# Attention products of a three-stage kernel: from high/low f32r pairs to plain f32 matmuls on 64-row and 64/32-column tiles of the array

## What is computed

```python
def phi(x):                                     # q and k, per head
    proj = x @ w_phi                            # 64 -> 128 features
    proj = proj - max(abs(proj), axis=-1)
    return concatenate([exp(proj), exp(-proj)])
kv, z = phi(k).T @ v, sum(phi(k), over tokens)
x = (phi(q) @ kv) / (phi(q) @ z + 1e-6)         # attention, no softmax matrix

xk, xr = mu_k*x + (1-mu_k)*x_prev, mu_r*x + (1-mu_r)*x_prev
y = sigmoid(xr @ w_r) * (relu(xk @ w_k)**2 @ w_v)          # "moe"

h = relu(y @ w_in)
out = (h * sigmoid(conv3(h))) @ w_out                      # "moe2"
```

## Time and profile before

| | us |
|---|---|
| median of 3 runs | 1486.46 (1486.41 to 1493.02) |
| profiled execution, first to last instruction (its span) | 1483.8 |
| TensorE matmuls busy | 1416.3 (95%) |
| VectorE busy / ScalarE busy | 818.5 / 797.9 (55% / 54%) |
| attention of the first batch, alone | 0 to 118 |
| seven iterations, attention with second stage | 118 to 997 |
| last second stage | 997 to 1057 |
| phase 2 | 1057 to 1484 |

### The profile page before, as it was taken

How to read it: one execution, slowest core, us unless ns; L and a number is a source line. 1 busy time by engine, 2 the same in 40 slices (tenths; PEclk the granted TensorE clock), 3 DMA queues, 4 the chain that set the end, 5 groups by cost and what they waited for, 6 DMA issues and landing times. The chain is left out here.

```text
span 1483.8 us, 26980 instructions
## 1 busy us (share of the span) xinstructions
PE 1416.3 (95%) x10240; PEld 1362.4 (92%) x10240; DVE 818.5 (55%) x1141; ACT 797.9 (54%) x1400; POOL 14.4 (1%) x20
## 2 busy tenths in 40 slices
PE   5778999999999999999999999999889999999998
PEld 5778999999999999999999999999879889988997
DVE  4565555554645564465555555554386468456653
ACT  4656674674666557466565746755244344344442
POOL 0000000000000000000000000000110000000000
PEclk9999999999999999999999999999999999999999
DMA  4412202211120221212122022121201110110101
GB/s 125 126 31 57 58 17 65 69 30 50 45 61 26 57 61 30 66 41 49 38 61 58 17 66 66 27 91 46 72 34 61 68 40 22 67 60 16 51 28 36
DMA packets 153461, 77.42 MB, mean 52 GB/s; under 512 B 131728, under 2 KB 140048, under 8 KB 152336
## 3 DMA queue, kind: packets, MB, share of 16 engines
q1 hardware_dynamic: 153360, 75.91, 18.5%
HBM read 56.71 MB, written 19.02 MB: 51 GB/s over the span
## 5 line engine op out<-in xcount | busy, mean ns | idle before, releaser
L512 PE MATMUL psm<-xk_hi,wk_hi 128*128 128x288 f32 x512 | 153.4, 300 | 16.5 <-DVE xk_lo L885 12.0
L1047 PE MATMUL psh<-y_hi,win_hi 128*128 128x288 f32 x512 | 154.0, 301 | 13.5 <-ACT h L1132 9.1
L1048 PE MATMUL psh<-y_lo,win_hi 128*128 128x288 f32 x512 | 152.5, 298 | 0.0
L512 PE MATMUL psm<-k_hi,wv_hi 128*128 128x288 f32 x512 | 152.1, 297 | 0.0
L1049 PE MATMUL psh<-y_hi,win_lo 128*128 128x288 f32 x512 | 151.9, 297 | 0.0
L512 PE MATMUL psm<-xk_lo,wk_hi 128*128 128x288 f32 x512 | 151.7, 296 | 0.0
L512 PE MATMUL psm<-xk_hi,wk_lo 128*128 128x288 f32 x512 | 151.2, 295 | 0.0
L512 PE MATMUL psm<-k_lo,wv_hi 128*128 128x288 f32 x512 | 151.1, 295 | 0.0
L512 PE MATMUL psm<-k_hi,wv_lo 128*128 128x288 f32 x512 | 150.8, 295 | 0.0
L890 DVE TENSOR_TENSOR k_lo<-square,k_hi 128x288 fp32r<-128x288 f32 x128 | 58.6, 458 | 156.1 <-ACT square L740 155.6
L1190 DVE SCALAR_TENSOR_TENSOR conv<-h,taps,conv 128x576 f32<-128x576 f32 x64 | 55.2, 863 | 141.7 <-ACT conv L1134 141.7
(11 more groups left out here) (157 smaller groups left out, 3832.2 us busy)
## 6 DMA issues: line engine op xcount, KB each, us to landing
den<-den_scr SPq DMA_DIRECT2D x64, 144.0 KB, 3.0
y_scr<-y SPq DMA_DIRECT2D x64, 144.0 KB, 2.6
y<-y_scr SPq DMA_DIRECT2D x8, 1152.0 KB, 5.7
qk_nat<-in_q SPq DMA_DIRECT2D x64, 128.0 KB, 2.5
qk_nat<-in_k SPq DMA_DIRECT2D x64, 128.0 KB, 2.5
v_nat<-in_v SPq DMA_DIRECT2D x64, 128.0 KB, 2.5
out<-rows SPq DMA_DIRECT2D x32, 256.0 KB, 2.0
stage<-in_moe_w_in SPq DMA_DIRECT2D x4, 512.0 KB, 3.2
```

What stands on the lines that cost most here:

```text
L512: return nc.tensor.matmul(o, lhsT, rhs, start=first, stop=last)
L1047: nc.tensor.matmul(o, wh, xh, start=first, stop=False, skip_group_check=True)
L1048: nc.tensor.matmul(o, wh, xl, start=False, stop=False, skip_group_check=True)
```

## The change

The host now lays out q and k transposed (128 rows of two heads, 576 tokens) and v by token block. The step `T`, all splits of attention operands and the diagonal weight block are gone. The products of the attention take plain `F32` operands that cover a part of the array:

- `QP`, `KP`: 64 rows, one head each: 10 matmuls, 128 feature columns. The heads alternate, heads 0 and 1 on rows 0 to 63 and 64 to 127.
- `P0`, `P1` replace `PA`, `PB`: one half of the tokens for both heads: 2 plain matmuls of 64 rows over 288 columns, then 2 f32r matmuls of 64 rows for the maxima.
- `KV`: the same 20 matmuls, 65 columns. One copy out instead of four.
- `DEN` (new): the denominators apart, 8 matmuls with a single stationary column, on PSUM rows 0, 32, 64 and 96.
- `NUM` replaces `NA`, `NB`: 8 matmuls with 64 stationary columns, head 0 on PSUM rows 0 to 63, head 1 on 64 to 127.
- The denominators go out by four DMAs instead of one, and VectorE adds their two parts before it inverts them.

```diff
-PE_NS = {"T": 1100, "QP": 1600, "KP": 1600, "M": 500, "PA": 1000, "PB": 1000, "KV": 2200, "NA": 1500,
-         "NB": 1500, "K": 1480, "K-": 1110, "K+": 370, "R": 1480, "V-": 1480, "V": 1480}
+PE_NS = {"QP": 1100, "KP": 1100, "M": 550, "P0": 800, "P1": 800, "KV": 2240, "DEN": 1000, "NUM": 1950,
+         "K": 1590, "K-": 1190, "K+": 400, "R": 1590, "V-": 1590, "V": 1590}
-FILL_NS = {"QP": 1500, "M": 1500, "PA": 3000, "T": 2200}
+FILL_NS = {"QP": 2200, "M": 1600, "P0": 3500, "P1": 2600}
...
+        steps += [(s, p) for s in ("KP", "M", "EK", "P0", "KV", "P1", "DEN", "NUM")]
+        steps += [("QP", p + 1)] if p + 1 < PAIRS else []
...
         def project(i, p, a):
...
+            for n in range(TT):
+                for h, t in ((0, (n - 1) % TT), (1, (n + 1) % TT)):
+                    own, b = slice(D * h, D * h + D), place(h, t)
...
+                    last = mm(ps[:, F * b:F * b + F], qk[own, p % 2, i, P * t:P * t + P], phi[own, :], True, True)
...
+        def feature_rows(n, p, a):
...
+            for h in range(2):
+                own = slice(D * h, D * h + D)
+                mm(ps1[:, BANK * h:BANK * h + HALF], phi[own, :], qk[own, p % 2, 0, cols], True, False)
+            for h in range(2):
+                own = slice(D * h, D * h + D)
+                last = mm(ps1[:, BANK * h:BANK * h + HALF], pick[own, :], max_rows[own, cols], False, True)
...
+        def sum_den(p, a):
...
+            for n in range(2):
+                cols = slice(HALF * n, HALF * n + HALF)
+                for h in range(2):
+                    for e in range(2):
+                        row = 32 * (2 * h + e)
+                        last = mm(ps[row:row + 1, BANK * (1 + n):BANK * (1 + n) + HALF], kvz[:, h, e, D:D + 1], q_exp[:, e, h, cols],
+                                  True, True)
...
+        def attend(p, a):
...
+            for n in range(2):
+                cols = slice(HALF * n, HALF * n + HALF)
                 for e in range(2):
+                    for h in range(2):
+                        last = mm(ps1[D * h:D * h + D, BANK * n:BANK * n + HALF], kvz[:, h, e, 0:D], q_exp[:, e, h, cols],
+                                  e == 0, e == 1)
```

More of the change, by code:

```diff
@@ L80, in before @@
             return [(s, p - 1)] if p else []
[L82 to L88, removed]
+        steps += [("M", p)] + before("RC") + [("P0", p), ("EK", p)] + ahead("QP")
+        steps += [("KV", p), ("P1", p)] + before("DV") + ahead("KP") + [("DEN", p), ("NUM", p)]
+        if last:
+            steps += [("XK", 2, 0), ("HK", 2, 0), ("LK", 2, 0), ("RC", p)]
+            steps += [("XR", 2, 0), ("HR", 2, 0), ("LR", 2, 0), ("DV", p)]
     return steps + [(s + w, 2, 1) for w in "KR" for s in "XHL"]
@@ L138, in iteration @@
             s, p = step[:2]
-            if not (ran_ahead and step in (("T", 0), ("QP", 0), ("KP", 0))):
+            if not (ran_ahead and step in (("QP", 0), ("KP", 0))):
                 emit(step)
@@ L356, in await_bank @@
         if before < 0 and first_of(batch):
[L357 removed]
+            eng.wait_ge(den_copied, PAIRS)
             return
@@ L386, in load_qk @@
         def load_qk(p, a):
-            await_(sp, turned, PAIRS, a, p)
             reg, off = a
-            for i, (src, loaded) in enumerate(((q, q_loaded), (k, k_loaded))):
-                b = src[off] if reg is None else src[reg + off]
-                for h in range(2):
-                    sp.dma_start(qk_nat[:, i, 0:4, D * h:D * h + D],
-                                 b[2 * p + h, 0:4 * P, :].rearrange("(t s) d -> s t d", s=P)).then_inc(loaded, 16)
-                sp.dma_start(qk_nat[0:TAIL, i, 4, :].rearrange("s (h d) -> s h d", h=2),
-                             b[2 * p:2 * p + 2, 4 * P:S, :].rearrange("h s d -> s h d")).then_inc(loaded, 16)
+            await_(sp, features, H, a, 2 * (p - 1))
+            sp.dma_start(qk[:, p % 2, 0, 0:S], q[off, p] if reg is None else q[reg + off, p]).then_inc(q_loaded[p % 2], 16)
+            await_(sp, k_projected, PAIRS, a, p - 1)
+            sp.dma_start(qk[:, p % 2, 1, 0:S], k[off, p] if reg is None else k[reg + off, p]).then_inc(k_loaded[p % 2], 16)
         def load_v(p, a):
@@ L498, in _ @@
                                 pattern=[[-1, P]], channel_multiplier=1).then_inc(ident_ready, 1)
-        for n, (part, h) in enumerate([(0, 0), (0, 1), (1, 0), (1, 1)]):
+        for n, row in enumerate((0, 1, D, D + 1)):
             pool.wait_ge(pick_made, 1 + n)
-            nc.gpsimd.affine_select(out=pick_f[:, h, :], in_=pick_f[:, h, :], compare_op=ALU.not_equal, fill=-1.0,
-                                    base=-(2 * part + h), pattern=[[0, F]], channel_multiplier=1).then_inc(pick_made, 1)
+            nc.gpsimd.affine_select(out=pick_f, in_=pick_f, compare_op=ALU.not_equal, fill=-1.0,
+                                    base=-row, pattern=[[0, F]], channel_multiplier=1).then_inc(pick_made, 1)
         pool.wait_ge(zeroed, 1)
@@ L592, in attend @@
                 for e in range(2):
-                    last = three(ps1[:, BANK * n:BANK * n + HALF], (kvz_hi[:, h, e, :], kvz_lo[:, h, e, :]),
-                                 (hi[:, e, cols], lo[:, e, cols]), e == 0, e == 1)
+                    for h in range(2):
+                        last = mm(ps1[D * h:D * h + D, BANK * n:BANK * n + HALF], kvz[:, h, e, 0:D], q_exp[:, e, h, cols],
+                                  e == 0, e == 1)
             last.then_inc(attended, 1)
@@ L723, in copy_num @@
[L723 to L730 removed]
+            await_(act, attended, PAIRS, a, p)
@@ L749, in split_mix @@
                 await_(act, r_done, 2 * XT, m, XT * n)
-            if which and n == 2 and m[0] is None and m[1] == -1:
-                act.wait_ge(attended, H)
             await_(act, mixed, 2 * XT, m, XT * n + fs.stop)
```

325 lines of the change are left out of this document (126 added, 199 removed).

## The result

| | before | after |
|---|---|---|
| median of the runs, us | 1486.62 (1486.41 to 1493.02, 4 runs) | 1419.55 (1415.0 to 1425.01, 4 runs) |
| span of the profiled execution, us | 1483.8 | 1415.8 |
| first batch alone, until the second stage's long stretch | 118.3 | 102.9 |
| one iteration, mean of seven | 125.6 | 118.2 |
| last second stage and phase 2 | 486.3 | 485.8 |

A forecast was written before the change was run, and what follows sets the result against it. Seven iterations were taken as bound by TensorE's matmul stream, the first batch by a chain of hand-overs. Sum: 1486.5 - 39 + 18 - 13 + 5 = 1457.5, stated as 1457 us; range 1388 to 1522, the forecast's own 1445 to 1472.

The forecast's parts named there:

- parts replaced, 28 pairs, if tiles cost what their records need: Attention steps on TensorE in the iterations: 8.6 us a pair against 10.0, 39 us less over 28 pairs.
- changes of form in the iterations: TensorE switching between whole-array and partial-tile matmuls: 294 times at 0.06 us, 18 us more.
- new waits in the iterations: `KP` waiting for maxima, `DEN` for exponentials: 0.25 us at three places in each iteration, 5 us more.
- first batch: Attention running alone at the start: earlier start and shorter hand-over chain, less its changes of form, 13 us less.
- Pairs of neighbours overlap, never more, whatever the number of tiles: Tiled attention steps on TensorE: overlap only in pairs, so `DEN` and `NUM` 2.2 us each, 8.6 us a pair.
- first rival: Tiled steps: records queued for one tile don't hold up another; 6.4 us a pair instead of 8.6, 1392 us; chance 0.22.
- The estimate of 1.3 us for `DEN` by that page: `DEN`: its 3.9 us of records divided by the skill's four-row-tile factor 3.07, giving 1.3 us.
- second rival: All 336 changes of form empty the array: 0.23 us each instead of 0.06, 57 us more, 1514 us; chance 0.25.
- The nearest row taken for the price: Trace's plain-to-f32r change after `KV`, 0.06 us more than the pace, taken as the price of a change of form.
- The price of a plain record: Plain f32 matmul records on TensorE: 0.245 us for 288 columns, 0.11 us for 128.
- `KV` paced by its loads: `KV`: weight loads of 128 columns, two for each product, set its pace; one column less changes nothing.
- Work taken off ScalarE and VectorE buys nothing: Seven iterations: the matmul stream is the bound, so removing six large splits a pair gains nothing there.

The follow-up runs named there:

- experiment 1: Changed kernel with `QP`, `KP`, `DEN` and `NUM` issuing all products of one tile, then all of the next, instead of alternating: 1510.0 us, ratio 1.0154.
- experiment 2: Changed kernel with one of twelve f32r matmuls in each of the 64 second-stage tiles `R` covering only 64 rows: 1442.05 us, ratio 0.9697.
- experiment 6: Changed kernel with `KV`'s 128 stationary columns in two pieces of 64, each on its own column tile: 1367.82 us, ratio 0.9197.
- experiment 4: Changed kernel with three useless splits a pair added back, ScalarE copy and VectorE difference waiting for each other: 1468.53 us, ratio 0.9883.
- experiment 5: Same useless operations as experiment 4 on the changed kernel, but ScalarE and VectorE not waiting for each other: 1443.08 us, ratio 0.9705.
- experiment 7: Changed kernel with `KV`'s 128 stationary columns in four pieces of 32, each on its own column tile: 1384.94 us, ratio 0.9321.
- experiment 8: Changed kernel with the first batch's weight-piece loads issued ahead of the loads of q and k: 1424.66 us, ratio 0.9580.
- experiment 10: Changed kernel with `KV` in pieces of 64, weight pieces loaded ahead of q and k and hung on `QP`, `P1`, `NUM`: 1362.21 us, ratio 0.9161.

## Why the prediction came out less than half as large

The direction held and the time lies in the range, but the forecast's own range, 1445 to 1472, missed it. Term by term, in us; measured values are sums over the starts of the two traces (the long stretch holds the projections and transposes of 27 pairs and the other steps of 28; 9.86, 7.35 and 6.30 are its sums shared out over 28):

| term | forecast | measured |
|---|---|---|
| parts replaced, 28 pairs, if tiles cost what their records need | -39 | 28 x (9.86 - 6.30) = -100 |
| changes of form in the iterations | +18 | +50 |
| new waits in the iterations | +5 | -2 |
| first batch | -13 | -15.5 |
| the rest | 0 | -0.5 |

- **The step that failed is the overlap.** "Pairs of neighbours overlap, never more, whatever the number of tiles" was derived from the order of the records. `DEN` alone refutes it: 1.08 us, not 2.2, which is 31 us over 28 pairs. The two-tile steps do not pay a start slot either: `NUM` is 2.09 us for eight slots of 0.242, which is 1.94, and a change. That their whole times, changes included, still came out near the forecast's (`NUM` 2.09 for 2.2, a projection 1.31 for 1.21, `P0` 0.82 for 0.87) is luck: the slot stood in for a change of form that was priced too low. The first rival, "each tile keeps its own order", had 6.4 us a pair for this, and `DEN` at 1.0. Experiment 1 shows how far it goes, to about four records of a tile.
- **The Trainium skill** (TensorE: Matmul & The Clock Gate, Part 3) has matmuls start and end in program order. The trace disagrees for the starts of different tiles: in experiment 1 a later record of one tile starts before earlier queued ones of the other. The estimate of 1.3 us for `DEN` by that page was nearer than the forecast, and still above the 1.08; its factor of 3.07 is one for four row tiles, and `DEN` runs on four column tiles.
- **Changes of form were under-priced as well**, with the opposite sign. The 50 us are 29 inside the tiled steps (28 x (7.35 - 6.30)), 4 in `KV` and the maxima and 16 in the second stage: 0.17 us for each of 294, where 0.06 was taken. Experiment 2 gives 0.20 for 64-row tiles. This is the second rival's mechanism near its upper price. It stayed on the fast side since the first rival came true too: 1392 + 336 x 0.11 is 1429, and 1422 without the 7 us of waits that did not come, near the 1419.6 measured. The nearest row taken for the price, from plain to f32r, was no change of form at all; in the other direction such a change of type costs nothing (302.38 to 302.51). The Trainium skill (TensorEngine Tiling, Key Properties) says that a change of the tiling mode drains the engine. The trace agrees that a change has a price, 0.09 us at the entry and the rest where a load of 64 or 128 columns stands behind it; that the engine empties it does not show, since the record ahead of `DEN` ends, as modelled, at 286.76 + 0.29 = 287.05, after `DEN` has started at 286.99.
- **The price of a plain record held**: 0.242 us for 288 columns where 0.245 was taken, and 0.11 for 128. `KV` paced by its loads held too (experiment 6).
- **The first batch** came out right by luck, from errors that cancel. The first `KV` starts at 18.8, not 22, as TensorE had only the load of `w_phi` to wait for. The undisturbed period is 15.9 us, not 17.4 (the last of three), but the first two are 20.7 and 20.0, with the pauses behind the weight pieces and the half clock, which I had not looked for. From the last `KV` to the long stretch it is 2.7 us longer than before, where the forecast had no term.
- **The waits** did not come: in the iterations neither `KP` nor `DEN` waits. They are close, though: experiment 4 brings the one forth, experiment 6 the other. The wait that did grow, of the turned maxima for the copy of the numerator (4.5 to 9.1 us, first batch), is one that the prediction did not name.
- **"Work taken off ScalarE and VectorE buys nothing"** in the iterations holds to 0.9 us an iteration (experiment 5), as long as the two engines are not coupled. Experiments 4 and 5 do not show that the old splits cost anything in the old order, which had longer covers; that was not tried.

## What to carry to other kernels

Array tiles run side by side if their records alternate within a few; put the products of different tiles next to each other, and price each change between full and tiled form at up to 0.2 us, so that tiled steps are few and long. Where a matmul has few moving columns and many stationary ones, look at the weight load: two column tiles halved it here. And a step that gets faster was a cover for something: move other work into its place.

## What was not expected of the hardware

- A tile holds about four records, and the next holds up the other tiles' (experiment 1).
- The price of a change of form depends on the load behind it: 0.09 us in all with one stationary column, 0.05 more with 64, 0.10 more with 128 (0.20 for 64 rows of 128 columns, experiment 2).
- Four column tiles of 32 were worse than two of 64, only by 11.5 us of pauses inside 12 of 28 `KV` that no wait explains (experiment 7).
- The changed first batch fell to the 1.2 GHz level for some 31 us, and taking its pauses away moved those stretches rather than ending them (experiment 8); splitting `KV`'s columns and moving the weight pieces left, after the first clock entry at 24.5 us, only those after 75 us (experiment 10), which began in pauses of 4.68 and 3.58 us. What decides it inside a `KV` is open.
- A granted clock of 1.00 can mean that there is no reading: in the changed kernel the entries begin at 18.4 us, and the first projection, at 6.04, took 2.50 us, later 1.39.
